# Windowed attention with a routed expert layer: q and k transposed on the host, two heads on the partition halves, x gated in each step, expert 0 split earlier

## The reference

```python
# q, k, v: (4, 8, 576, 64); w_gate (512, 8), w_local (512, 1), w1 (8, 512, 1024), w2 (8, 1024, 512)
scores = (q @ k.T) / sqrt(64)
mask   = (0 <= rel < 32) for heads 0..3; (0 <= rel < 128) & (rel % 4 == 0) for heads 4..7
attn   = softmax(where(mask, scores, -1e9));  x = heads_side_by_side(attn @ v)     # (4, 576, 512)
logits = x @ w_gate;  local = sigmoid(x @ w_local)
# per batch, token by token: the expert is argmax(logits) at s == 0 or where local < 0.5,
# otherwise that of the token before
out = p[e] * (relu(x @ w1[e]) @ w2[e])            # p = softmax(logits)
gate = sigmoid(causal_conv_5_taps(out, conv_w));  result = (gate * (out @ w_val)) @ w_out
```

## Time and profile before

| | us |
|---|---|
| median of 3 runs | 661.99 (660.03 to 663.44) |
| span of the profiled execution | 663.2 |

### The profile page before, as it was taken

The page is one execution under the profiler, slowest core; times in us unless marked ns, Lnnn a source line. Parts: engine busy times, 40 slices in busy tenths (PEclk is TensorE's granted clock), DMA queues, the critical chain, the costliest instruction groups (busy, mean ns, idle before and its releaser), DMA issues.

```text
span 663.2 us, 12185 instructions
## 1 busy us (share of the span) xinstructions
PE 585.3 (88%) x3425; PEld 499.4 (75%) x3426; DVE 300.0 (45%) x888; ACT 226.4 (34%) x498; POOL 290.3 (44%) x209
## 2 busy tenths in 40 slices
PE   3896999989808699999999999999998487999988
PEld 2785979778706588887888888888886377898966
DVE  3583788848487111121121121121121559988510
ACT  2573565736000112122122122122122377674421
POOL 8150414200470664586235656375864625522210
PEclk9796999969557989999999999999998669899989
DMA  5858577491992699899597788779876421211112
GB/s 117 136 140 178 124 155 163 126 243 46 280 313 87 200 388 323 300 306 366 209 303 243 262 273 256 252 248 387 290 263 210 143 73 47 70 67 48 49 47 79
DMA packets 99357, 129.53 MB, mean 195 GB/s; under 512 B 46848, under 2 KB 57504, under 8 KB 99328
## 3 DMA queue, kind: packets, MB, share of 16 engines
q1 hardware_dynamic: 72240, 63.98, 32.8%
q0 software_dynamic: 19824, 52.98, 25.5%
q10 hardware_dynamic: 7264, 12.21, 5.4%
HBM read 105.80 MB, written 23.33 MB: 195 GB/s over the span
## 4 chain that ended last, share of the span: by engine, by line
PE 50%; SPq 16%; DMA 12%; DVE 8%; issue 7%; POOL 5%; ACT 2%; POOLq 0%; DVEq 0%; ACTq 0%
PE bank L1178 39%; SPq L356 11%; DMA w_high<-in_moe_w 4%; POOL w_low L565 3%; SPq L352 2%; PE bank L1383 2%; DMA x_sorted<-gathered 2%; DVE gate_acc L981 2%; PE bank L1251 2%; PE bank L1215 1%; POOL gathered L626 1%; DMA gathered<-x_tokens,token_idx 1%; DMA x_tokens<-x_dil 1%; PE bank L1261 1%; PE bank L1436 1%
## 5 line engine op out<-in xcount | busy, mean ns | idle before, releaser
L565 POOL TENSOR_TENSOR w_low<-stage,w_high 128x2048 f32 (+1 forms) x32 | 146.9, 4604 | 68.4 <-DMA stage<-in_moe_w 38.1
L1028 ACT ACTIVATE probs<-shifted,negmax 96x128 f32<-96x128 f32 x192 | 61.3, 390 | 58.0 <-DVE negmax L774 58.0
L1178 PE MATMUL bank<-w_high,h_high 128*128 x184 | 74.7, 406 | 3.7 <-DVE h_low L940 2.3
L1178 PE MATMUL bank<-w_high,x_high 128*128 x184 | 75.3, 409 | 2.7 <-DVE x_low L931 1.7
L1178 PE MATMUL bank<-w_high,x_low 128*128 x184 | 73.0, 397 | 0.0
L1178 PE MATMUL bank<-w_high,h_low 128*128 x184 | 72.8, 395 | 0.0
L1178 PE MATMUL bank<-w_low,x_high 128*128 x184 | 72.7, 395 | 0.0
L1178 PE MATMUL bank<-w_low,h_high 128*128 x184 | 72.3, 393 | 0.0
L1066 ACT CAST x_high<-bank 128x512 fp32r<-128x512 f32 x25 | 14.7, 587 | 156.1 <-PE bank L1348 148.9
L931 DVE TENSOR_TENSOR x_low<-bank,x_high 128x512 fp32r<-128x512 f32 x25 | 17.3, 691 | 111.3 <-ACT x_high L1066 104.1
L1080 ACT CAST h_high<-bank 128x1024 fp32r<-128x1024 f32 x25 | 25.4, 1015 | 120.1 <-PE bank L1383 120.1
(11 more groups left out here) (174 smaller groups left out, 1256.4 us busy)
## 6 DMA issues: line engine op xcount, KB each, us to landing
stage<-in_moe_w SPq DMA_DIRECT2D x32, 1024.0 KB, 7.5
w_high<-in_moe_w POOLq DMA_DIRECT2D x16, 2048.0 KB, 10.3
y_sorted<-y_sb ACTq DMA_DIRECT2D x25, 256.0 KB
x_sorted<-gathered SPq DMA_DIRECT2D x21, 256.0 KB, 13.3
x_in<-x_sorted ACTq DMA_DIRECT2D x21, 256.0 KB, 6.3
out<-o_sb SPq DMA_DIRECT2D x18, 256.0 KB
vwin<-in_v POOLq DMA_DIRECT2D x28, 128.0 KB, 3.3
q_rows<-in_q SPq DMA_DIRECT2D x16, 144.0 KB, 4.1
```

The costliest lines, as they stand in the source:

```text
L565: g.tensor_tensor(low, stage[:, c % 2, :], high.bitcast(F32), ALU.subtract).then_inc(split_done, 1)
L1028: a.activation(probs[:, j % 2, u, :], shifted[:, j % 2, u, :], ACT.Exp, bias=negmax[:, j % 2, u:u + 1], scale=-1.0).then_inc(exp_done, 1)
L1178: ins = mm(dst, l, r, start=first and i == 0, stop=last and i == 2)
```

## The change

The host now lays out q and k transposed, per pair of heads: head one on partitions 0 to 63, head two on 64 to 127, tokens of the strided heads in the order of their residues, keys padded with 32 zero columns in front. V comes as the key blocks of all tiles, with overlap, padding and the column of ones in place. Gates and conv weights come by partition.

- On the chip the transposes of q and k, their copies and `k_pair` are gone. qT, kT and vwin have two buffers each, one for even and one for odd batches. One DMA loads q of a pair, one k, one the V of a batch, all on SyncE's queue (the first q on ScalarE's); batches 0 and 1 are loaded at the start, batch b + 2 after batch b.
- `scores` are four products with 64 rows and 128 columns. Each head has a bank (0 and 1 in even steps, 2 and 3 in odd ones), and the transposed probs of the step are put into the first of the two. So `scores(j)` waits for the copy of the probs of step j - 2, and a transpose of probs for at least the first two exps.
- ScalarE issues per step: copy of transposed x of step s - 4, exps 0 and 1, copy of the probs of step s - 1, exps 2 and 3.
- Each step's output is transposed and multiplied with its k-block of the gates three and four steps later (banks 6 and 7). VectorE adds up the logits of pairs (`take_logits`). x is not read back; the logits of the strided heads are stored in pieces (36 bytes per token) and read back in token order (`lg_dram`, `lg_back`).
- POOL starts expert 0 when step 30 is normed, loads and splits it, then waits for all logits and for the last store of x_plain, and makes the routing constants after that. SyncE's raw loads of expert 0 lie between its stores of batch 2 and 3.
- Loops over batches are unrolled; `settle` is no longer called there.

```diff
+        qT = late("qT", [128, 2, PAIRS, SEQ], F32)
...
+        kT = hole("kT", [128, 2, PAIRS, WINDOW + SEQ], F32)
...
+            def load_pair(b, n, q_too=True):
+                if b >= 2:
+                    sp.wait_ge(scores_done, STEPS * (b - 2) + PAIR_STEPS * (n + 1))
+                if q_too:
+                    sp.dma_start(qT[:, b % 2, n, :], q_t[b, n]).then_inc(qk_loaded[b % 2][n], 16)
+                sp.dma_start(kT[:, b % 2, n, :], k_t[b, n]).then_inc(qk_loaded[b % 2][n], 16)
+
+            def load_v(b):
+                if b >= 2:
+                    sp.wait_ge(pv_done, STEPS * (b - 1))
+                sp.dma_start(vwin[:, b % 2].rearrange("p t h c -> p (t h c)"), v_win[b]).then_inc(v_loaded[b % 2], 16)
...
+                sp.wait_ge(lg_taken, STEPS * b + STEPS // 2)
+                lgs = batch_of(lg_dram, b)
+                dst = lgs.rearrange("o (j x r) c -> r j (o x) c", x=2, r=DIL // 2)
+                for t, m, r, j, n in QUERY_PIECES:
+                    sp.dma_start(dst[r, j:j + n, :, :],
+                                 lg_dil[m:m + n].rearrange("p (x t) c -> p t x c", x=2)[:, t]).then_inc(lg_stored, 16)
+                sp.wait_ge(lg_stored, 16 * len(QUERY_PIECES) * (b + 1))
+                if b > 0:
+                    sp.wait_ge(logits_ready, b)
+                sp.dma_start(lg_back[:, :, :], lgs.rearrange("o (t p) c -> p (o t) c", p=QB)).then_inc(lg_loaded, 16)
+
+            def store_plain(b):
+                sp.wait_ge(normed, STEPS * (b + 1))
+                sp.dma_start(batch_of(x_rows, b)[:, :, 0:MODEL // 2].rearrange("o (t p) c -> p (o t) c", p=QB),
+                             x_plain[:, :, :]).then_inc(plain_stored, 16)
...
+            load_pair(0, 0, q_too=False)
+            load_pair(0, 1)
+            load_v(0)
+            sp.dma_start(wg[:, :, :], w_gates.rearrange("p (k e) -> p k e", k=KD)).then_inc(small_loaded, 16)
+            sp.dma_start(convw[:, :, :], conv_t.rearrange("p (k t) -> p k t", k=KD)).then_inc(small_loaded, 16)
+            load_pair(0, 2)
+            load_pair(0, 3)
+            for n in range(PAIRS):
+                load_pair(1, n)
...
+            for b in range(BATCH):
+                store_dil(b)
+                if b == 2:
+                    load_raw(sp, 0, 0)
+                    load_raw(sp, 0, 1)
+                store_plain(b)
+                if b + 2 < BATCH:
+                    for n in range(PAIRS):
+                        load_pair(b + 2, n)
+                    load_v(b + 2)
+                if b == 2:
...
+                    sp.wait_ge(split_done, 2)
+                    load_raw(sp, 0, 3)
...
+            po.wait_ge(normed, 2 * STEPS + STEPS // 2)
+            load_high(0, 0, 0)
+            load_high(0, 0, 1)
+            for c in range(CHUNKS):
+                split(0, c, 0)
+            po.wait_ge(logits_ready, BATCH)
+            po.wait_ge(plain_stored, 16 * BATCH)
...
-            po.wait_ge(back_loaded, 16 * BATCH)
-            load_high(0, 0, 0)
-            load_high(0, 0, 1)
-            for c in range(CHUNKS):
-                split(0, c, 0)
...
+            def take_logits(m):
+
+                b, n, i = place_of(m)
+                dve.wait_ge(x_multiplied, m + 1)
+                part = (lg_plain if PAIR_HEAD[n] < 4 else lg_dil)[:, PW * i:PW * (i + 1), :]
+                got = bank[0:QB, 6 + m % 2, PW * QB:PW * QB + PW * LOGC].rearrange("p (t e) -> p t e", t=PW)
+                if n % 2 == 0:
+                    if n == 0 and i == 0 and b > 0:
+                        dve.wait_ge(lg_stored, 16 * len(QUERY_PIECES) * b)
+                    if n == 2 and i == 0 and b > 0:
+                        dve.wait_ge(logits_ready, b)
+                    d.tensor_copy(part, got).then_inc(lg_taken, 1)
+                else:
+                    dve.wait_ge(lg_taken, m - PAIR_STEPS + 1)
+                    d.tensor_tensor(part, got, part, ALU.add).then_inc(lg_taken, 1)
+                if n == PAIRS - 1 and i == PAIR_STEPS - 1:
+                    dve.wait_ge(lg_loaded, 16 * (b + 1))
+                    dve.wait_ge(lg_taken, m + 1)
+                    d.tensor_tensor(logits[:, NQ * b:NQ * (b + 1), :], lg_plain[:], lg_back[:], ALU.add
+                                    ).then_inc(logits_ready, 1)
...
+            for s in range(ALL_STEPS + 5):
+                if s >= 5:
+                    take_logits(s - 5)
+                if s < ALL_STEPS:
+                    mask_and_max(s)
+                if 2 <= s < ALL_STEPS + 2:
+                    norm(s - 2)
...
+            def exps(j, units):
+                if units[0] == 0 and j >= 2:
+                    act.wait_ge(probs_transposed, j - 1)
+                for u in units:
+                    act.wait_ge(shifted_done, UNITS * j + u + 1)
+                    a.activation(probs[:, j % 2, u, :], shifted[:, j % 2, u, :], ACT.Exp,
+                                 bias=negmax[:, j % 2, u:u + 1], scale=-1.0).then_inc(exp_done, 1)
+
+            def copy_probs(j):
+                act.wait_ge(probs_transposed, j + 1)
+                if j >= 2:
+                    act.wait_ge(pv_done, j - 1)
+                a.copy(probsT[:, j % 2, :], bank[:, 2 * (j % 2), 0:UNITS * QB]).then_inc(probs_copied, 1)
+
+            def copy_x(j):
+                act.wait_ge(x_transposed, j + 1)
+                if j >= 2:
+                    act.wait_ge(x_multiplied, j - 1)
+                a.copy(xT_sb[:, j % 2, :], bank[:, 6 + j % 2, 0:PW * QB]).then_inc(x_copied, 1)
...
+            for s in range(ALL_STEPS + 4):
+                if s >= 4:
+                    copy_x(s - 4)
+                if s < ALL_STEPS:
+                    exps(s, (0, 1))
+                if 1 <= s <= ALL_STEPS:
+                    copy_probs(s - 1)
+                if s < ALL_STEPS:
+                    exps(s, (2, 3))
...
+            def scores(j):
+                b, n, i = place_of(j)
                 if i == 0:
-                    if j == -2:
-                        pe.wait_ge(first_loaded, 16 * len(QUERY_PIECES))
...
+                    pe.wait_ge(probs_copied, j - 1)
...
+                    for hh in range(2):
+                        rows = slice(hh * HD, (hh + 1) * HD)
+                        ins = mm(bank[0:QB, 2 * (j % 2) + hh, w * KB:(w + 1) * KB],
+                                 qT[rows, b % 2, n, t * QB:(t + 1) * QB],
+                                 kT[rows, b % 2, n, t * QB:t * QB + KB], start=True, stop=True)
                 ins.then_inc(scores_done, 1)
...
+            def transpose_probs(j):
+                for u in range(UNITS):
+                    pe.wait_ge(exp_done, UNITS * j + max(u + 1, PW))
+                    ins = tr(bank[:, 2 * (j % 2), u * QB:(u + 1) * QB], probs[:, j % 2, u, :], ident[0:QB, 0:QB])
+                ins.then_inc(probs_transposed, 1)
...
+            def transpose_out(j):
+                b, n, i = place_of(j)
                 if j >= 2:
...
+                h = PAIR_HEAD[n]
+                for w in range(PW):
+                    src = (x_plain if h < 4 else x_dil)[:, PW * i + w, (h % 4) * HD:(h % 4 + 2) * HD]
+                    ins = tr(bank[:, 6 + j % 2, w * QB:(w + 1) * QB], src, ident[0:QB, 0:QB])
                 ins.then_inc(x_transposed, 1)
...
+            def gate_logits(j):
+
+                b, n, i = place_of(j)
+                if j == 0:
+                    pe.wait_ge(small_loaded, 32)
+                pe.wait_ge(x_copied, j + 1)
+                for w in range(PW):
+                    at = PW * QB + w * LOGC
+                    ins = mm(bank[0:QB, 6 + j % 2, at:at + LOGC], xT_sb[:, j % 2, w * QB:(w + 1) * QB],
+                             wg[:, PAIR_HEAD[n] // 2, :], start=True, stop=True)
+                ins.then_inc(x_multiplied, 1)
...
+            for s in range(ALL_STEPS + 5):
+                if s < ALL_STEPS:
+                    scores(s)
+                if 1 <= s <= ALL_STEPS:
+                    transpose_probs(s - 1)
+                if 2 <= s <= ALL_STEPS + 1:
+                    times_v(s - 2)
+                if 3 <= s <= ALL_STEPS + 2:
+                    transpose_out(s - 3)
+                if s >= 4 and s < ALL_STEPS + 4:
+                    gate_logits(s - 4)
```

More of the change, by code:

```diff
@@ L760, in mask_and_max @@
-            def mask_and_max(b, j):
-                at = STEPS * b + j
-                n, i = split_step(j % STEPS)
-                dve.wait_ge(scores_done, at + 1)
+                dve.wait_ge(pv_done, m + 1)
+                d.tensor_scalar(den[:], o[:, :, HD], EPS, None, ALU.add).then_inc(den_ready, 1)
+                dve.wait_ge(den_ready, 2 * m + 1)
+                d.reciprocal(rden[:], den[:]).then_inc(den_ready, 1)
+                if b > 0 and i == 0 and n == 0:
+                    dve.wait_ge(dil_stored, 16 * len(QUERY_PIECES) * b)
@@ new lines, in norm @@
+                if b > 0 and i == 0 and n == 2:
+                    dve.wait_ge(plain_stored, 16 * b)
```

(44 more changed lines are left out.)

343 lines of the change are left out of this document (65 added, 278 removed).

## The result

| | us | measured beside it, kernel before |
|---|---|---|
| median of 4 runs | 672.92 (671.08 to 673.90) | 661.03 (660.03 to 663.44) |
| ratio after / before | 1.017, 95% interval 1.013 to 1.021 | |
| span of the profiled execution | 670.9 | 663.2 |

The account below looks back on a forecast made before the run. Before the experts, TensorE's work, load waits and routing stalls were taken to bound the kernel; then a 2.63 us scores loop. 663.2 - 35.5 (earlier routing) - 11.4 (split stalls) = 616.3 us span, 615.1 median; range 597 to 632.

Parts of the forecast that it names:

- 47 x 2.63 us: Attention: 47 steps of 2.63 us from scores to scores, through mask, two exps and probs copy; TensorE's own work 2.36.
- slower than before: the clock: Rival, attention: added wait idles TensorE, clock stays at 1.2 GHz, 4.72 us per step, 98 us more, 713; chance 0.03.
- point of decision: Attention, clock rival: it decides from the point where a step takes 3.63 us.
- two products at once: Rival, scores: both heads' products overlap; load floor 0.65 us gives 10.3 us less, 604.8; fully halved 594; chance 0.30.
- first scores: Start of attention: scores begin at 6.0 us instead of 11.65, masks being ready ahead of the loads.
- last norm: End of attention: 6.0 + 2 + 47 x 2.63 + 5.9 = 137.5 us, against 168.5 before.
- last norm to routing: After attention: VectorE waits for the x_plain store and POOL's constants, 7.7 us, so routing starts at 145.2.
- routing, shortened by: Routing: three VectorE operations no longer stand for POOL's splits of expert 0, giving back 11.4 us.
- from the experts on: Experts to the end: the change touches nothing there, so as long as before.
- load floor of 0.65 us: Scores if two products overlap: eight loads, priced from V's records, take at least 0.65 us; loop then 2.41.
- The reciprocal: Rival, batch 3 of attention: VectorE's reciprocal blocks beside splits, four times, 11 us more, 626; chance 0.08.
- VectorE's operations there read PSUM, all but the reciprocal: Batch 3 of attention: claim that VectorE is untouched by the splits moved there, which were costed at nothing.

Follow-up runs that it names:

- e2: Changed kernel with each scores product reading all 128 rows, so scores sum both heads and the output differs: 616.0 us.
- e5: Changed kernel with scores on 128 rows, the other head's half of q zeroed, output right, one q buffer per pair: 615.5 us, ratio 0.934.
- e1: Changed kernel with six dense products of 128 rows and 512 columns on TensorE ahead of the first scores: 681.9 us, 668.0 before beside it.
- e3: Changed kernel with all four scores products on the lower 64 rows, so both heads get the first head's scores: 713.1 us.
- e10: e7 plus the dense burst of e1 ahead of the first scores: 606.2 us, ratio 0.916.
- e6: e5 with routing constants made at GpSimd's start and the wait for the x_plain store moved to VectorE: 607.8 us, ratio 0.925.
- e11: Kernel before with its scores products on the first 64 rows only, so the output differs: 760.5 us, 663.7 before beside it.
- e7: Changed kernel with early routing constants and one unused product of 128 rows and 128 columns per step: 600.5, 691.2, 694.4 and 694.8 us.
- e4: Changed kernel with the four 64-row scores products executed twice per step, same output: 624.7 us.
- e12: Changed kernel with early routing constants and four more unread transposes of 96 rows per step: 706.8 us.

## Why the prediction was wrong

**The step that failed** is the term 47 x 2.63 us, the loop from scores to scores. All its parts were priced from rows at the upper clock, and attention ran at the lower one: 3.98 us from the fifth step on, with TensorE busy throughout instead of waiting for ScalarE's copy. At the upper clock the loop, its path and its length were right (2.62 us, e2). The prediction had this case as its last rival, "slower than before: the clock", with a chance of 0.03. That rival's mechanism was the lower level through all of attention, its price the step's sum at half speed. Its point of decision was right: it decides from a step of 3.63 us on, and the step is 3.98. Its price was 4.72 x 47 mainly because I gave it the scores of one product at a time, 1.74 us; with the overlap of the other rival (0.30) they take 1.10, the sum is 3.98, and the result 673 instead of 713. The two rivals came true together, which the list did not have.

Two things in its weighing failed. I tied it to idle time ("the added wait makes TensorE idle"), while the trace after has almost no idle time and the lower clock all the same, and e2, with the idle time, has the upper one. And the row against it, 553 to 559 us busy for 3.73 of 6 us at clock 1.00, is of the stage behind the experts, the convolution and the output. What the change altered, that the scores' products fill 64 rows instead of 128, occurs nowhere in the trace of before at any load that could have been compared; a row without it could not speak against it. The trace of before even held a warning. Behind the last attention step, after a pause of 1.1 us, TensorE has only transposes of x and products of nine columns, and the table has:

```profile
168.50:180.70 12.20, 11.71 (x72) 11.35 (x72) 3.56 (x8) 0.00 (x0) 5.35 (x3) 0.50 1.02 323
```

TensorE is busy for 11.71 of 12.20 us, and the granted clock is 0.50: a busy TensorE and the lower level go together there already. And the first line of the earlier trace rows, used only for its DMA rate, has it busy for 4.00 of 4 us at 0.63.

The Trainium skill ("TensorE: Matmul & The Clock Gate", "Why this matters for your kernels") names idle gaps between bursts as what drops the clock. The rule holds in e5 (3.9 us idle, then the lower level) and does not cover the changed kernel, where the level is low with TensorE busy without a gap (40.00 of 40 us, and the same in e1 at 0.50).

**Point by point.**

| step of the prediction | forecast | measured |
|---|---|---|
| loop, scores to scores | 2.63 us | 3.98; at the upper clock 2.62 (e2) |
| first scores | 6.0 | 5.12 |
| last norm | 137.5 | 195.9; 136.9 (e2) |
| last norm to routing | 7.7 | 6.7 |
| routing, shortened by | 11.4 | 12.4 |
| from the experts on | as before, 449.7 | 447.8 |
| span | 616.3 | 670.9; 614.4 (e2) |

Routing before: 180.70 to 213.5, 32.8 us; after: 202.68 to 223.10, 20.4. The term that was mis-sized is the loop. From the first scores (5.12) to the last (186.88) are 181.8 us for a forecast 47 x 2.63 = 123.6, so 58.2 more; the first four steps have less work and are shorter than 3.98. The other terms: the start 2.9 less (5.12 for 6.0 + 2), from the last scores to the last norm 3.2 more (9.1 for 5.9, the lower clock again), and the three rows of the table behind the last norm 3.9 less: 616.3 + 58.2 - 2.9 + 3.2 - 3.9 = 670.9.

Of the other rivals, two products at once is true (e3), and its load floor of 0.65 us was too high: eight records take 0.61 at the upper clock (e10). The reciprocal did not block.

**What the change does for itself.** It removes the load stalls and the q and k transposes (e2 and e5: 616, 615), and moves the x tail and the splits out of the routing. It also takes away half of the rows on which scores worked, and for that alone pays 57 us (672.9 against 616.0, on two chips; 64 us if each is taken against the kernel before beside it, 661.0 and 668.0). Made with full rows it gains 6.6% (e5), and 7.5% with the constants made early (e6).

**Said wrongly though it cost little.** "VectorE's operations there read PSUM, all but the reciprocal" overlooked the sum of logits, once a batch. In four of the profiled executions it met a split. The reciprocal was never blocked: 173 to 174 ns, 48 times in the changed kernel.

## To carry to other kernels

When an edit cuts TensorE's work into products with fewer rows, ask first at which clock the rest of the step will run, and hold no row of full-height products against the doubt: a chance of a few hundredths for a factor of two needs a row of the same kind of work. In the trace after, compare the duration of a product that the change left alone (here V, 0.65 and 1.23 us) before reading busy shares, for at the lower clock an engine looks perfectly busy. Where heads of 64 are to be packed on the partition halves, try the zero-padded 128-row form beside it; here it was 57 us faster with twice the nominal work (e5).

## What was not expected of the hardware

- By its durations TensorE stayed at 1.2 GHz through attention, busy for 189.8 of 195.9 us, with scores on 64 rows, and was at 2.4 GHz from the third step on with the same products on 128 rows (step 3.98 and 2.62 us). Scores on 64 instead of 128 rows in the kernel before: from 663.7 to 760.5 us (e11).
- Under one and the same load (e7) both levels were seen, 600.5 and 691 to 695 us; with a dense burst ahead four executions of four took 604 to 612 us (e10, another chip). What the chip measures to choose was not found out here; the runs show outcomes only. More rows brought the upper level (e2, e5), more products of 64 rows did too (e4), more transposes did not (e12).
- Two 64-row products on different halves overlap: four (eight records) took 1.10 us and, all on one half, 1.95, at the lower clock. The Trainium skill ("TensorEngine Tiling (Array Packing)", Overview) gives up to 2x; this is 1.8x.
